# Local attention with four buffers in place of three, and TensorE's attention program written as a loop over four units

## What is computed

```
for c in range(nc):                       # 24 chunks of 32 positions
    q_c = q[:, :, c_start:c_end]
    k_full = concat([mem_k, k[l_start:r_end]])        # up to 8 + 56 keys
    v_full = concat([mem_v, v[l_start:r_end]])
    scores = scale * q_c @ k_full.T
    a = exp(scores - max(scores)); a = a / (sum(a) + 1e-9)
    out[:, :, c_start:c_end] = a @ v_full
```

## Time and profile before

| | |
|---|---|
| median of three runs | 848.15 us (841.01 to 848.68) |
| the profiled execution | 842.02 us, its span 840.3 us |
| attention, from the start to the last normalised unit | 0 to 151.6 us |
| threshold search, to the first weights gathered | 151.6 to 200 us |
| experts and last block | 200 to 840 us |
| TensorE busy, whole span | 714.3 us, 85% |
| VectorE busy | 578.6 us, 69% |
| ScalarE busy | 344.9 us, 41% |
| GpSimd busy | 332.2 us, 40% |
| instructions fetched by DMA | 0.88 MB in 54 packets, and 0.24 MB in 29 |

### The profile page before, as it was taken

The page is one execution under the profiler, slowest core; times in us unless marked ns, Lnnn a source line. Parts: engine busy times, 40 slices in busy tenths (PEclk is TensorE's granted clock), DMA queues, the critical chain, the costliest instruction groups (busy, mean ns, idle before and its releaser), DMA issues.

```text
span 840.3 us, 17631 instructions
## 1 busy us (share of the span) xinstructions
PE 714.3 (85%) x6838; PEld 616.9 (73%) x6838; DVE 578.6 (69%) x2167; ACT 344.9 (41%) x553; POOL 332.2 (40%) x243
## 2 busy tenths in 40 slices
PE   4679587411699899999999999999999999999993
PEld 3546465200598789898888989898988979898882
DVE  3456466888687886878798778769877886832140
ACT  3446455101222651473256136515723561473170
POOL 2000000797741760574067137515721750574001
PEclk9989788755699999999999999999999999999997
DMA  9777674422401320331132023113302320331000
GB/s 260 225 220 243 223 229 141 152 76 91 147 1 52 112 76 26 113 114 51 51 101 100 27 88 114 59 44 113 113 26 62 114 76 26 113 114 50 1 13 37
DMA packets 24275, 83.91 MB, mean 100 GB/s; under 512 B 3968, under 2 KB 4032, under 8 KB 24192
## 3 DMA queue, kind: packets, MB, share of 16 engines
q0 software_dynamic: 14208, 50.34, 17.7%
q1 hardware_dynamic: 9984, 32.45, 12.2%
HBM read 70.19 MB, written 12.58 MB: 99 GB/s over the span
## 4 chain that ended last, share of the span: by engine, by line
PE 61%; POOL 9%; DVE 9%; issue 9%; DMA 7%; ACT 3%; SPq 1%; POOLq 0%; DVEq 0%; ACTq 0%
PE bank L518 16%; PE bank L520 15%; PE bank L519 15%; POOL wl L1300 6%; DMA raw<-w,w_idx 5%; PE bank L461 3%; PE banks L443 3%; PE bank L418 2%; PE bank L428 2%; PE bank L454 2%; DMA vr<-v_in 2%; POOL raw L1294 2%; DVE hits L963 1%; DVE z L1092 1%; DVE hot_a L963 1%
## 5 line engine op out<-in xcount | busy, mean ns | idle before, releaser
L1300 POOL TENSOR_TENSOR wl<-raw,wh 128x1024 fp32r<-128x1024 f32 x60 | 146.2, 2438 | 19.2 <-ACT wh L736 17.7
L1294 POOL DMA_INDIRECT raw<-w,w_idx x60 | 65.4, 1091 | 158.9 <-DVE w_idx L1012 121.2
L736 ACT ACTIVATE wh<-raw 128x1024 fp32r<-128x1024 f32 x60 | 63.4, 1056 | 84.9 <-DMA raw<-w,w_idx 84.6
L518 PE MATMUL bank<-xh,wh 128*128 128x384 f32 x256 | 90.8, 355 | 3.4 <-POOL wl L1300 3.2
L518 PE MATMUL bank<-hh,wh 128*128 128x384 f32 x256 | 90.1, 352 | 0.0
L519 PE MATMUL bank<-xl,wh 128*128 128x384 f32 x256 | 86.7, 339 | 0.0
L520 PE MATMUL bank<-xh,wl 128*128 128x384 f32 x256 | 86.5, 338 | 0.0
L520 PE MATMUL bank<-hh,wl 128*128 128x384 f32 x256 | 86.0, 336 | 0.0
L519 PE MATMUL bank<-hl,wh 128*128 128x384 f32 x256 | 85.9, 336 | 0.0
L518 PE MATMUL bank<-wout_h,uh 128*128 128x512 f32 x192 | 78.5, 409 | 0.2
L518 PE MATMUL bank<-win_h,yh 128*128 128x512 f32 x192 | 77.3, 403 | 0.0
(11 more groups left out here) (180 smaller groups left out, 1736.1 us busy)
## 6 DMA issues: line engine op xcount, KB each, us to landing
unit<-qk_in SPq DMA_DIRECT2D x24, 768.0 KB, 6.3
vr<-v_in SPq DMA_DIRECT2D x48, 130.0 KB
x_rows<-x_sb SPq DMA_DIRECT2D x24, 256.0 KB, 3.7
raw<-w_in POOLq DMA_DIRECT2D x4, 512.0 KB, 4.2
raw<-w_out POOLq DMA_DIRECT2D x4, 512.0 KB, 3.8
raw<-w,w_idx POOLq DMA_INDIRECT x60, 4.2
vr<-v_mem SPq DMA_DIRECT2D x24, 32.5 KB
gath<-x_rows,ids POOLq DMA_INDIRECT x24, 3.5
```

Of the source, the lines that this page charges most:

```text
L518: nc.tensor.matmul(bank, stat_h, mov_h, start=first, stop=False)
L736: nc.scalar.activation(wh[:, c % WCH, :], stage(s, c), ACT.Copy).then_inc(w_hi, 1)
L1294: gp.indirect_dma_start(stage(s, c), None, table, bass.IndirectOffsetOnAxis(ap=w_idx[:, c % WCH:c % WCH + 1], axis=0))\
L1300: gp.tensor_tensor(wl[:, c % WCH, :], stage(s, c), wh[:, c % WCH, :].bitcast(F32), ALU.subtract)\
```

## The change

A constant DEEP = 4 takes the place of the 3 that was written in the buffers' sizes, in the semaphores' lists, in the modulos and in the distances of the waits. So `unit`, `vr` and `x_sb` have four buffers, a load waits for the unit four back, four units are loaded ahead of the first store, and the V of the memory is loaded for the first four units of a batch (the ring has one more buffer to fill).

TensorE's list is no longer 27 written-out steps. Steps 0 to 3 are written out, then comes a loop that runs five times over a body of four steps (units 4 to 23), then the last three steps are written out. In the body the unit's number is a register (`b * DEEP + r`), so the waits compare a semaphore with a register's value, and all waits are there in each step. The other engines' lists stay written out.

```
-RING = 3 * CPT
+DEEP = 4
+RING = DEEP * CPT
-        qk_loaded = [sem(f"qk_loaded{i}") for i in range(3)]
+        qk_loaded = [sem(f"qk_loaded{i}") for i in range(DEEP)]
...
-        unit = sb("unit", [P, 3, QW + KW], F32, attn)
+        unit = sb("unit", [P, DEEP, QW + KW], F32, attn)
...
-        x_sb = sb("x_sb", [P, 3, HP, 2, D], F32, attn)
+        x_sb = sb("x_sb", [P, DEEP, HP, 2, D], F32, attn)
...
-            n = u // 3
-            return 64 * (n // 2 + 1) + 32 * ((n + 1) // 2) - (32 if u == NT else 0)
+            return sum(64 if n % TPB < DEEP and n < NT else 32 for n in range(u % DEEP, u + 1, DEEP))
...
-            engine.wait_ge(v_loaded[(u + 1) % 3], v_count(u + 1))
-            if u >= 3:
-                engine.wait_ge(pv_ps, u - 2)
+            engine.wait_ge(v_loaded[(u + 1) % DEEP], v_count(u + 1))
+            if u >= DEEP:
+                engine.wait_ge(pv_ps, u - DEEP + 1)
...
             def load_qk(u):
-                if u >= 3:
-                    sp.wait_ge(scores_ps, u - 2)
-                sp.dma_start(unit[:, u % 3, :], qk_in[u, :, :]).then_inc(qk_loaded[u % 3], 16)
+                if u >= DEEP:
+                    sp.wait_ge(scores_ps, u - DEEP + 1)
+                sp.dma_start(unit[:, u % DEEP, :], qk_in[u, :, :]).then_inc(qk_loaded[u % DEEP], 16)
             def load_v(u):
-                if u >= 3:
-                    sp.wait_ge(pv_ps, u - 2)
+                if u >= DEEP:
+                    sp.wait_ge(pv_ps, u - DEEP + 1)
...
-            load_qk(2)
-            load_v(2)
-            load_qk(3)
+            for u in range(2, DEEP):
+                load_qk(u)
+                load_v(u)
+            load_qk(DEEP)
             for u in range(NT):
-                if u + 4 < NT:
-                    load_qk(u + 4)
-                if u + 3 <= NT:
-                    load_v(u + 3)
-                store(u, u)
+                if u + DEEP + 1 < NT:
+                    load_qk(u + DEEP + 1)
+                if u + DEEP <= NT:
+                    load_v(u + DEEP)
+                store(u)
...
-            def scores(u, r):
-                pe.wait_ge(qk_loaded[r % 3], 16 * (u // 3 + 1))
-                if u >= 2:
+            def scores(u, r, n):
+                pe.wait_ge(qk_loaded[r], 16 * n)
+                if not (isinstance(u, int) and u < 2):
                     pe.wait_ge(shifted, u - 1)
-                if u >= 4:
+                if not (isinstance(u, int) and u < 4):
                     pe.wait_ge(gate_sb, u - 3)
...
+            def step(i, r, n):
+
+                known = isinstance(i, int)
+                if not known or i < NT:
+                    scores(i, r, n)
+                if not known or 1 <= i <= NT:
+                    probs_T(i - 1, (r - 1) % DEEP)
+                if not known or i >= 3:
+                    gate(i - 3, (r - 3) % DEEP)
+                if not known or 2 <= i <= NT + 1:
+                    x_T(i - 2, (r - 2) % DEEP)
+                if not known or 1 <= i <= NT:
+                    values(i - 1, (r - 1) % DEEP)
...
-            for i in range(NT + 3):
-                if i < NT:
-                    scores(i, i % TPB)
-                if 1 <= i <= NT:
-                    probs_T(i - 1, (i - 1) % TPB)
-                if i >= 3:
-                    gate(i - 3, (i - 3) % TPB)
-                if 2 <= i <= NT + 1:
-                    x_T(i - 2, (i - 2) % TPB)
-                if 1 <= i <= NT:
-                    values(i - 1, (i - 1) % TPB)
+            for i in range(DEEP):
+                step(i, i, 1)
+            with pe.Fori(1, NT // DEEP) as b:
+                for r in range(DEEP):
+                    step(b * DEEP + r, r, b + 1)
+            for i in range(NT, NT + 3):
+                step(i, i % DEEP, 0)
...
                 if n is not None:
-                    ve.wait_ge(x_stored[r % 3], 16 * n)
-                    ve.wait_ge(xT_ps, u - 2)
+                    ve.wait_ge(x_stored[u % DEEP], 16 * n)
+                    ve.wait_ge(xT_ps, u - DEEP + 1)
```

More of the change, by code:

```diff
@@ L176, in build @@
         small_in = sem("small_in")
-        qk_loaded = [sem(f"qk_loaded{i}") for i in range(3)]
-        v_loaded = [sem(f"v_loaded{i}") for i in range(3)]
-        x_stored = [sem(f"x_stored{i}") for i in range(3)]
+        qk_loaded = [sem(f"qk_loaded{i}") for i in range(DEEP)]
+        v_loaded = [sem(f"v_loaded{i}") for i in range(DEEP)]
+        x_stored = [sem(f"x_stored{i}") for i in range(DEEP)]
         scores_ps = sem("scores_ps")
@@ L344, in next_front @@
                 engine.wait_ge(v_loaded[0], v_count(0))
-            engine.wait_ge(v_loaded[(u + 1) % 3], v_count(u + 1))
-            if u >= 3:
-                engine.wait_ge(pv_ps, u - 2)
+            engine.wait_ge(v_loaded[(u + 1) % DEEP], v_count(u + 1))
+            if u >= DEEP:
+                engine.wait_ge(pv_ps, u - DEEP + 1)
             own, after = slice(64 * a, 64 * a + FRONT), slice(64 * a + CHUNK, 64 * a + CHUNK + FRONT)
-            s = CPT * (u % 3)
+            s = CPT * (u % DEEP)
             if s + CPT < RING:
@@ L365, in load_qk, with store @@
             def load_qk(u):
-                if u >= 3:
-                    sp.wait_ge(scores_ps, u - 2)
-                sp.dma_start(unit[:, u % 3, :], qk_in[u, :, :]).then_inc(qk_loaded[u % 3], 16)
+                if u >= DEEP:
+                    sp.wait_ge(scores_ps, u - DEEP + 1)
+                sp.dma_start(unit[:, u % DEEP, :], qk_in[u, :, :]).then_inc(qk_loaded[u % DEEP], 16)
             def load_v(u):
-                if u >= 3:
-                    sp.wait_ge(pv_ps, u - 2)
-                slots = slice(CPT * (u % 3), CPT * (u % 3) + (CPT if u < NT else 1))
+                if u >= DEEP:
+                    sp.wait_ge(pv_ps, u - DEEP + 1)
+                slots = slice(CPT * (u % DEEP), CPT * (u % DEEP) + (CPT if u < NT else 1))
                 for a in range(2):
-                    if u % TPB < 3 and u < NT:
+                    if u % TPB < DEEP and u < NT:
                         sp.dma_start(vr[64 * a + 64 - MEM:64 * a + 64, slots, :, :].rearrange("p c h d -> p (c h d)"),
-                                     v_mem[u // TPB, a, :, :]).then_inc(v_loaded[u % 3], 16)
+                                     v_mem[u // TPB, a, :, :]).then_inc(v_loaded[u % DEEP], 16)
                     own = vr[64 * a:64 * a + CHUNK, slots, :, :].rearrange("p c h d -> p (c h d)")
-                    sp.dma_start(own, v_in[u, a, :, 0:own.shape[1]]).then_inc(v_loaded[u % 3], 16)
-            def store(u, r):
+                    sp.dma_start(own, v_in[u, a, :, 0:own.shape[1]]).then_inc(v_loaded[u % DEEP], 16)
+            def store(u):
                 sp.wait_ge(x_ready, u + 1)
-                sp.dma_start(x_dram[u * P:u * P + P, :], x_sb[:, r % 3, :, :, :].rearrange("p a b d -> p (a b d)"))\
-                  .then_inc(x_stored[r % 3], 16)
+                sp.dma_start(x_dram[u * P:u * P + P, :], x_sb[:, u % DEEP, :, :, :].rearrange("p a b d -> p (a b d)"))\
+                  .then_inc(x_stored[u % DEEP], 16)
             load_qk(0)
@@ L390, in _ @@
             load_v(1)
-            load_qk(2)
-            load_v(2)
-            load_qk(3)
+            for u in range(2, DEEP):
+                load_qk(u)
+                load_v(u)
+            load_qk(DEEP)
             for u in range(NT):
-                if u + 4 < NT:
-                    load_qk(u + 4)
-                if u + 3 <= NT:
-                    load_v(u + 3)
-                store(u, u)
-            for i in range(3):
-                sp.wait_ge(x_stored[i], 16 * NT // 3)
+                if u + DEEP + 1 < NT:
[4 more added lines that the diff above has]
+            for i in range(DEEP):
+                sp.wait_ge(x_stored[i], 16 * NT // DEEP)
         @block.tensor
         def _(pe):
-            def scores(u, r):
-                pe.wait_ge(qk_loaded[r % 3], 16 * (u // 3 + 1))
-                if u >= 2:
+            def scores(u, r, n):
+                pe.wait_ge(qk_loaded[r], 16 * n)
+                if not (isinstance(u, int) and u < 2):
                     pe.wait_ge(shifted, u - 1)
-                if u >= 4:
+                if not (isinstance(u, int) and u < 4):
                     pe.wait_ge(gate_sb, u - 3)
                 pe.sem_inc(pe_past, 1)
-                q, k = q_of(r % 3), k_of(r % 3)
+                q, k = q_of(r), k_of(r)
                 for hp in range(HP):
@@ L435, in values @@
                     pe.wait_ge(v_next[a], u + 1)
-                if u >= 1:
+                if not (isinstance(u, int) and u < 1):
                     pe.wait_ge(x_ready, u)
@@ L445, in values @@
                                 pT[rows, r % 2, hp, CHUNK * c:CHUNK * (c + 1)],
-                                vr[rows, CPT * (u % 3) + c, hp, :], start=True, stop=True)
+                                vr[rows, CPT * r + c, hp, :], start=True, stop=True)
                 mm.then_inc(pv_ps, 1)
@@ L454, in x_T @@
```

(22 more changed lines are left out.)

## The result

The changed kernel takes 820.84 us in the median of four runs (817.24 to 824.59), the one before 848.35 us on the same chip (841.01 to 848.68). The ratio is 0.9716, with a 95% interval of 0.9681 to 0.9751: 2.8% faster. In a later comparison the same two kernels gave 819.29 and 843.94 us, 0.9704 (0.9667 to 0.9741). The profiled execution took 817.24 us, its span 815.5.

The account below looks back on a forecast made before the run. No engine fills the attention; TensorE stops for late 256-instruction program blocks. 842.0 - 23 (units 8 to 23) + 1 (units 0 to 7) = 820, put at 822 us; own range 806 to 832, widened to 806 to 861.

Parts of the forecast that it names:

- The decisive step: TensorE's loop body, about five blocks, stays in its instruction memory, so units 8 to 23 fetch nothing; little better than even.
- the 10 to 13 forecast: Sign of being right: TensorE's instruction queue brings 10 to 13 packets in the attention, not 27.
- 15 steps from unit 8 to unit 23: Attention's looped steps: 4.5 us each, 67.5 us against 90.7, so 23 us gone.
- The "unbroken" step: One TensorE attention step without a stop in the kernel before, 4.00 us, used to price the looped steps.
- Register work: In the loop body each of twelve waits needs its own instruction and arithmetic: 0.3 us a step, 4.5 us.
- rival B: Register work of 1.5 us a step eats the gain, 844 us; chance 0.16 with other ends near today's time.
- DMA floor: Attention's transfers take 4.2 us a unit, nearly TensorE's step; cost 0.2 us a step, 3 us.
- Rival C: DMA takes over in the attention, steps of 5.2 us, 830 us; chance counted within the forecast's 0.57.
- Units 0 to 7: Start of the attention, blocks still fetched behind a deeper load queue: between 3 us lost and 2 won, 1 lost.
- Tail and sequel: Work after unit 23's scores stays 8.85 us, and w_idx moves one for one with the attention's end: both cost 0.
- its cover: GpSimd's 50.4 us preparation stays hidden before w_idx: cost 0, or 1 to 2 us if the cover is gone.
- The range: Whole kernel: the forecast's own range 806 to 832 us, widened to 861 to leave out no more than 2 in 10.

Follow-up runs that it names:

- 9.2 blocks: Changed kernel with eight steps written out and a loop of two passes over a body of eight steps; 849.25 us, ratio 1.0037.
- the unaligned 6.93: Kernel before, three buffers kept, TensorE's steps as a loop of three passes over six steps, not placed on a block's boundary; 840.34 us, ratio 0.9932.
- fewer bytes: Changed kernel, but from unit 8 on each load of queries and keys brings only half its columns; 813.64 us, ratio 0.9625.
- the run made for it: Changed kernel with unit 3's queries, keys and V loads put off at the start; 821.34 us, ratio 0.9719.
- the loop from unit 3: Changed kernel with three steps written out ahead, the loop over units 3 to 22, unit 23 in the tail; 816.75 us, ratio 0.9670.
- the loop alone on a good place: Kernel before with three buffers and a loop over six steps, its body starting on a 256-instruction block's boundary; 831.68 us, ratio 0.9849.

## Why the prediction was right

The forecast was 822 us with blocks kept, at a chance of 0.57; measured were 820.84. The decisive step, that TensorE keeps a body of five blocks, no row could settle beforehand, and the prediction took it at little better than even. The 9 packets, the empty q8 line, and the two bodies that did not fit (9.2 blocks, and the unaligned 6.93) settle it. The body has 1,184 instructions and touches five blocks, not six or seven, hence 9 packets in place of the 10 to 13 forecast. That the forecast came within 1.2 us is partly luck: the steps from unit 8 on gained 7 us more than forecast, and what the first eight units and the experts' part lost beyond it, 3 us and 2.6 us, took most of that back.

The size of a block can be read more directly than from 27 packets. Counted over TensorE's recorded instructions, the twelve "issue" stops of over 1 us in the attention before fall behind instruction 449, 705, 1,473, 1,986, 2,241 and so on to 5,826, each 449 plus a multiple of 256, within one. The changed kernel's four fall behind 449, 705, 1,474 and 1,985, and it has no "issue" stop of that length from unit 8 on.

- **15 steps from unit 8 to unit 23.** Predicted 67.5 us, 4.5 each. Measured 116.34 - 56.01 = 60.33, 4.02 each. The scores of unit 23 began at 142.63 before; the 142.72 of the earlier trace rows is where the chain enters them. So 90.65 - 60.33 = 30.3 us are gone, not 23. The "unbroken" step of 4.00 us was no floor: in the loop it is 3.70. That step's scores ran 1.05 us, behind a step at the lower clock, and its `values` 0.94 us; in the loop they take 0.85 and 0.86. A written-out step can be as short: with four buffers and no loop, unit 5's scores follow unit 4's by 37.51 - 33.81 = 3.70 us. So the step was too long a sample, and crossing into a new block does not always cost time.
- **Register work.** Predicted 0.3 us a step, since each of twelve waits was taken to need arithmetic of its own. The trace of the loop has eight register instructions of 32 to 50 ns in four steps, one of them in most steps, issued while matmuls are queued, and none of the idle time at the groups' boundaries that rival B needs. What the loop costs is the jump, 0.5 us in four steps, 1.9 us over the four jumps back. Rival B is out.
- **DMA floor.** Predicted 0.2 us a step, 3 us. Units 18 to 22 took 4.44 - 3.70 = 0.7 us more each, 3.7 us in all, 0.5 us of it the jump before unit 20. The size was about right and the shape was not: the floor cost nothing as long as the loads had a lead, and then all of it at once. Rival C is where the kernel now stands. As the steps fell to 3.7 us, the transfers became what sets the end: the data queue held all engines for 84.9% of 125.2 us, 4.4 us a unit. With fewer bytes these five steps took 19.1 us, and with an earlier unit 8 unit 23 began no sooner.
- **Units 0 to 7.** Predicted 1 us lost, measured 56.01 - 51.98 = 4.0 (2.1 in the other execution). The mechanism that I named, a deeper queue in front of the first blocks, is not shown by the run made for it. Where unit 8 began 5.5 us sooner, in the loop from unit 3, unit 23 did not, so this loss matters little here.
- **Tail and sequel.** Predicted 0 for both. The tail is 8.83 us against 151.57 - 142.63 = 8.94. That is not sure to stay so: it was 11.0 us in the loop from unit 3 and 11.2 with the fourth load put off, both with VectorE's last copies slow (3.57 and 3.74 us, against 1.60) while GpSimd worked on w_in, which the prediction did not look for. GpSimd waited 5.32 us for w_idx, so its cover held. The attention ended 26.4 us sooner, w_idx came 199.35 - 171.98 = 27.4 us sooner, and the span shrank by 24.8 us. The 2.6 us between the last two are in the experts' part, where no instruction was changed: from w_idx on it took 643.5 us against 640.9. The granted clock over the 60 us from 240 was 0.94, and over the like stretch of before 0.97, but that does not explain it: in the other profiled execution of the changed kernel it was 0.97 there, and the part took 643.6 us. Over all profiled executions it took 640.2 to 645.0 us; no run isolates why.
- **The range.** Its own low end, 806 us, does not follow from the terms named: 4.0 us a step and 2 us won at the start give 842.0 - 30.7 - 2 = 809.
- **The halves.** The prediction gave the fourth buffer a part of the gain without pricing it alone. Alone it gives nothing that can be measured (1.0011), the loop alone on a good place gives 0.9849, both give 0.9716. So the buffer pays only with the loop. The likely reason, argued and not isolated: as long as TensorE stands for its instructions, it doesn't matter how many units lie ready.

Still open: why the block behind the unaligned body of six pushed out the oldest only at the end of the second pass. At the end of the first it was not fetched at all: after the packet at 68.28 us none came until 100.62, and then two within 0.7 us. Open too is what made the first eight units 2 to 4 us longer, and whether the loop from unit 3 is faster by its 0.3 to 0.5% or not.

## What to carry to other kernels

Idle "issue" time in the middle of a run of matmuls, with 16 KB packets of an instruction queue landing just before it ends, is program text that is late. Here a loop whose body touches at most seven blocks of 256 TensorE instructions, with the one behind it the eighth, removed it from the second pass on, and where the body starts in a block decided. The fourth buffer was worth nothing before that, and after it the transfers were the next bound, so look how much of the DMA engines' time is left before pricing the gain. Before moving work off a chain, look for the second path that ends at the same time.

## What the hardware showed that I had not expected

- TensorE keeps eight blocks of 256 instructions, oldest out first, as these runs bound it: bodies of 1,184 and (aligned) 1,775 instructions were not fetched again; the unaligned 1,775, which touch eight blocks, ran once from what was kept and were fetched again in the third pass, and 2,365 were at once. The Trainium skill, page "Advanced Engine Details and Errata", section "ISA Cache", has both 128 KB for TensorE and "Only 2 cache lines!"; the runs agree with the first and not with the second.
- A jump back to a kept block cost TensorE 0.39 to 0.50 us, of which 0.21 to 0.24 us is the compare-and-branch; one to a lost block cost 4.07 us in the body of eight and 6.48 us in the unaligned body of six.
- Waits on registers showed no cost beside waits on constants: a looped step with twelve of them took 3.70 us, and so did a written-out one with four buffers and no loop.
